# Second FFN's input: blocked loads, gate scaling on GpSimd and 32x32 turns on VectorE in place of TensorE products with the identity

## The reference

```python
def _moe_ref(x, w_gate, w1, w2):            # x: 3072 rows of 512
    logits = x @ w_gate                     # 8 experts
    expert_idx = np.argmax(logits, axis=1)
    probs = softmax(logits); gate_w = probs[np.arange(N), expert_idx]
    for e in range(8):                      # rows of expert e
        out[mask] = gate_w[mask, None] * (np.maximum(x[mask] @ w1[e], 0.0) @ w2[e])

def _moe2_ref(x, w_in, w_out, a, b):        # 512 -> 2048 -> 512
    h = x @ w_in
    P = a[0] + a[1] * h + a[2] * h**2 + a[3] * h**3
    Q = 1.0 + np.abs(b[0]) * np.abs(h) + np.abs(b[1]) * h**2
    return (P / (Q + 1e-06)) @ w_out
```

## Time and profile before

| | before |
|---|---|
| median of 3 runs | 1113.38 us (1112.99 to 1115.29) |
| the profiled execution | 1118.07 us, span 1116.4 us |
| TensorE busy | 1088.4 us, 97% |
| VectorE busy | 921.7 us, 83% |
| ScalarE busy | 593.2 us, 53% |
| GpSimd busy | 259.6 us, 23% |
| granted TensorE clock | 0.996 |

### The profile page before, as it was taken

One profiled execution on the slowest core, in us unless ns is written; L12 is line 12 of the kernel. 1 busy time (PEld: TensorE's weight loads), 2 busy tenths in 40 slices (PEclk: granted clock), 3 DMA queues, 4 the chain that ended last, 5 costly groups with the idle time before them and its releaser, 6 DMA issues.

```text
span 1116.4 us, 19594 instructions
## 1 busy us (share of the span) xinstructions
PE 1088.4 (97%) x5911; PEld 878.1 (79%) x5912; DVE 921.7 (83%) x1844; ACT 593.2 (53%) x1060; POOL 259.6 (23%) x191
## 2 busy tenths in 40 slices
PE   6999999899999999999999999999999999999997
PEld 4777777678888888888787888888888888888885
DVE  5788888759898989898859979977986986987975
ACT  6878888322323232323257556556655665655663
POOL 1022111255756666564300002002001002000101
PEclk9999999999999999999999999999999999999999
DMA  8999771288877978796531010010001002000000
GB/s 200 251 288 262 175 204 50 72 249 298 273 237 262 313 224 282 252 294 219 179 98 38 1 39 38 1 39 38 0 31 45 0 0 72 5 0 10 29 1 38
DMA packets 155754, 142.52 MB, mean 128 GB/s; under 512 B 106160, under 2 KB 122032, under 8 KB 154672
## 3 DMA queue, kind: packets, MB, share of 16 engines
q0 software_dynamic: 27584, 92.48, 24.2%
q1 hardware_dynamic: 127824, 49.19, 17.6%
q10 hardware_dynamic: 288, 0.13, 0.0%
HBM read 118.70 MB, written 23.32 MB: 127 GB/s over the span
## 4 chain that ended last, share of the span: by engine, by line
PE 70%; DVE 8%; DMA 1%; ACT 1%; issue 1%; POOL 0%; POOLq 0%; ACTq 0%; DVEq 0%
PE bank L1177 23%; PE bank L1178 23%; PE bank L1179 23%; DVE bank L1704 1%; DVE poly L1800 1%; DVE poly L1798 1%; PE bank L1249 1%; DVE poly L1813 1%; DVE gl L1822 1%; DMA routed_x<-xt,slot_now 0%; DVE quot_a L1792 0%; DVE quot_a L1816 0%; DVE quot_a L1807 0%; DVE w_lo L1768 0%; DVE quot_b L1816 0%
## 5 line engine op out<-in xcount | busy, mean ns | idle before, releaser
L1704 DVE STREAM_TRANSPOSE bank<-hbuf 32x256 f32<-32x256 f32 x464 | 211.5, 456 | 28.7 <-ACT hbuf L781 22.2
L499 POOL TENSOR_TENSOR w_lo<-stage,w_hi 128x2048 fp32r<-128x2048 f32 x32 | 147.6, 4614 | 66.4 <-DMA w_hi<-in_moe_w_dram 32.6
L1177 PE MATMUL bank<-w_hi,gh 128*128 128x512 f32 x384 | 150.5, 392 | 0.3 <-DVE gl L1822 0.3
L1177 PE MATMUL bank<-x2Th,w_hi 128*128 128x512 f32 x384 | 149.5, 389 | 0.5 <-DVE poly L1800 0.5
L1179 PE MATMUL bank<-w_hi,gl 128*128 128x512 f32 x384 | 149.5, 389 | 0.0
L1178 PE MATMUL bank<-w_lo,gh 128*128 128x512 f32 x384 | 149.4, 389 | 0.0
L1179 PE MATMUL bank<-x2Th,w_lo 128*128 128x512 f32 x384 | 149.4, 389 | 0.0
L1178 PE MATMUL bank<-x2Tl,w_hi 128*128 128x512 f32 x384 | 149.4, 389 | 0.0
L635 POOL DMA_INDIRECT out_dram<-stage,ids x24 | 29.6, 1235 | 510.1 <-ACT stage L895 494.4
L1177 PE MATMUL bank<-w_hi,xTh 128*128 (+1 forms) x240 | 97.1, 405 | 0.8 <-DVE xTl L1610 0.8
L1178 PE MATMUL bank<-w_lo,xTh 128*128 (+1 forms) x240 | 94.2, 392 | 0.0
(11 more groups left out here) (228 smaller groups left out, 2225.8 us busy)
## 6 DMA issues: line engine op xcount, KB each, us to landing
w_hi<-in_moe_w_dram POOLq DMA_DIRECT2D x32, 1024.0 KB, 7.8
stage<-in_moe_w_dram POOLq DMA_DIRECT2D x32, 1024.0 KB, 8.2
routed_y<-ybuf SPq DMA_DIRECT2D x31, 256.0 KB, 3.4
xg<-routed_x SPq DMA_DIRECT2D x122, 64.0 KB, 5.1
x<-routed_y SPq DMA_DIRECT2D x6, 1056.0 KB, 5.1
kraw<-in_k_dram SPq DMA_DIRECT2D x24, 256.0 KB, 4.8
qraw<-in_q_dram SPq DMA_DIRECT2D x24, 256.0 KB, 4.5
vraw<-in_v_dram SPq DMA_DIRECT2D x24, 256.0 KB, 3.9
```

The costliest lines, as they stand in the source:

```text
L499: pool.tensor_tensor(w_lo[:, at:at + CH], stage[:, c % 2, :], w_hi[:, at:at + CH].bitcast(F32), ALU.subtract).then_inc(chunk_ready, 1)
L1177: pe.matmul(dst, lhs_hi, rhs_hi, start=first, stop=False)
L1704: ins = dve.transpose(HB_ps[k][r * QD:(r + 1) * QD, :, q % 2 * QD:(q % 2 + 1) * QD], rows)
```

## The change

- `load_x2` now issues nine transfers a group in place of one. Four bring 32 partitions of `x2` each: partition 32a + n holds, for each of 16 blocks b of 32 rows, 128 numbers of row 32b + n. Four bring the logits to the same four quarters, so each gate is computed in all four. One brings the token numbers (`idf`). The load of the next group waits for the turns on VectorE and for the token numbers to be taken over.
- `moe_y` writes `ybuf` in another order of its columns, so that the four quarters of a stored row are what the four quarters of partitions need.
- The gate work runs on 128 partitions by 16 by 8 rather than by 4 by 8.
- The multiplication by the gate is one instruction over 128x2048 with the gate as second operand. For group 0 VectorE does it (`scale_first`), for groups 1 to 5 GpSimd (`scale_x2`), ahead of the scatter of the group before.
- TensorE's turns go. VectorE turns each half with one 32x32-block transpose of 128x1024, for group 0 into `x2f` (where `x2Tl` will stand), for the others at the ends of steps 5 and 6 into the unused half of `stage`. `x2_high` and `x2_low` read there.
- At the end of the expert stage ScalarE does `gate_exp(0)` after `moe_h` and `moe_x`, and VectorE does `moe_ht` of the last but one tile before the gate work.
- `up` waits for `poly_ready` from step 0 on in later groups, since the turn that held that wait is gone.

The core of the diff:

```diff
+        x2t = [stage[:, k, CH // 2:CH].rearrange("p (j n) -> p j n", j=2) for k in range(2)]
+        x2f_half = [x2f[:, 2 * k:2 * k + 2, :] for k in range(2)]
             def load_x2(g):
-                sp.dma_start(x2[:, :, :], ys[ds(g * G * P, G * P), :].rearrange("(j p) n -> p j n", p=P)).then_inc(x2_in, 16)
+                rows = ds(g * G * P, G * P)
+                for a in range(4):
+                    own = slice(a * QD, (a + 1) * QD)
+                    sp.dma_start(glog[own, :, :], ys[rows, DM:TOK].rearrange("(b n) e -> n b e", n=QD)).then_inc(x2_in, 16)
+                    sp.dma_start(x2[own, :, :], ys[rows, a * P:(a + 1) * P].rearrange("(b n) c -> n b c", n=QD)).then_inc(x2_in, 16)
+                sp.dma_start(idf[:, :, :], ys[rows, TOK:RW].rearrange("(j p) o -> p j o", p=P)).then_inc(x2_in, 16)
...
-            with pool.Fori(0, NG) as g:
+            def scale_x2(g):
+                pool.wait_ge(g_step, 3 * (g + 1))
+                settle(pool)
+                pool.tensor_tensor(x2[:, :, :], x2[:, :, :],
+                                   gate[:, 3, :].rearrange("p (b o) -> p b o", o=1).broadcast_to([P, G * P // QD, P]),
+                                   ALU.mult).then_inc(x2_scaled, 1)
...
+            with pool.Fori(0, NG - 1) as g:
+                scale_x2(g + 1)
+                scatter(g)
+            scatter(NG - 1)
...
-            gate_exp(0)
-            act_tile(MT - 2)
+            moe_h(MT - 2); moe_x(MT - 1); gate_exp(0); moe_y(MT - 3); moe_ht(MT - 2)
             moe_h(MT - 1)
-            x2_high(0, 0, first_ps)
             end_ht(2, hLh)
+            x2_high(0, 0, x2f_half[0])
+            x2_high(0, 1, x2f_half[1])
+            moe_y(MT - 2)
             split_high(0)
             split_high(1)
-            moe_y(MT - 2)
-            x2_high(0, 1, first_ps)
...
-            turn_x2(0, 0, first_ps)
             turn_end_h(MT - 1)
             moe_down(MT - 2, off_down, e_down)
-            turn_x2(0, 1, first_ps)
             moe_down(MT - 1, off_last, e_last, YL_ps, hLh, hLl)
...
-                if p >= 2:
+                if p >= 2 or later(g):
                     pe.wait_ge(poly_ready, n - 1)
...
-                    if p == PAIRS - 1 and not last:
-                        turn_x2(g + 1, 0, pair_ps[0])
                     if p >= 2:
                         down(g, p - 2, again)
-                if not last:
-                    turn_x2(g + 1, 1, pair_ps[1])
...
-                for j in range(G):
-                    ins = dve.tensor_scalar(x2[:, j, 0:DM], x2[:, j, 0:DM], gate[:, 3, j:j + 1], None, ALU.mult)
-                ins.then_inc(x2_scaled, 1)
+            def turn_x2(g, k, dst):
+                dve.wait_ge(x2_scaled, g + 1)
+                dve.transpose(dst.rearrange("p j (b n) -> p j b n", n=QD),
+                              x2[:, :, 2 * k * QD:2 * (k + 1) * QD].rearrange("p b (j n) -> p j b n", n=QD)).then_inc(x2_turned, 1)
...
                     if not last and p == 4:
-                        gate_scale(g + 1)
+                        gate_sum(g + 1)
+                    if not last and p in (5, 6):
+                        turn_x2(g + 1, p - 5, x2t[p - 5])
```

More of the change, by code:

```diff
@@ L166, in build_program @@
         x2_at = free[1]
-        x2 = over("x2", [P, G, RW])
+        x2 = over("x2", [P, G * P // QD, P])
+        glog = over("glog", [P, G * P // QD, E])
+        gate = over("gate", [P, 4, G * P // QD])
+        idf = over("idf", [P, G, RW - TOK])
         xSh, x2_at = place("xSh", [P, KB, P], F32R, x2_at)
@@ L170, in build_program @@
         x2Th = over("x2Th", [P, KB, G * P], F32R)
+        x2f, _ = place("x2f", [P, KB, G * P], F32, free[1])
         x2Tl = over("x2Tl", [P, KB, G * P], F32R)
@@ L1728, in _, with gate_sum @@
             turn_rows(MT - 1, 0, MT // 2 + 1)
+            per_row = lambda k, n: gate[:, k, :].rearrange("p (b o) -> p b o", o=1).broadcast_to([P, G * P // QD, n])
             def gate_shift(g):
[L1732 to L1733 removed]
+                dve.wait_ge(x2_in, 144 * (g + 1))
+                dve.tensor_reduce(gate[:, 0, :], glog[:, :, :], AX.X, ALU.max).then_inc(g_shift, 1)
                 dve.wait_ge(g_shift, 2 * g + 1)
[L1735 to L1740, removed]
+                dve.tensor_tensor(glog[:, :, :], glog[:, :, :], per_row(0, E), ALU.subtract).then_inc(g_shift, 1)
+                dve.tensor_copy(ids[:, 1, :], idf[:, :, 0]).then_inc(ids_next, 1)
+            def gate_sum(g):
                 dve.wait_ge(g_exp, g + 1)
@@ L1746, in gate_scale, with scale_first @@
                 dve.reciprocal(gate[:, 3, :], gate[:, 2, :]).then_inc(g_step, 1)
-                dve.wait_ge(g_step, 3 * g + 3)
-                for j in range(G):
-                    ins = dve.tensor_scalar(x2[:, j, 0:DM], x2[:, j, 0:DM], gate[:, 3, j:j + 1], None, ALU.mult)
-                ins.then_inc(x2_scaled, 1)
+            def scale_first():
+                dve.wait_ge(g_step, 3)
+                dve.tensor_tensor(x2[:, :, :], x2[:, :, :], per_row(3, P), ALU.mult).then_inc(x2_scaled, 1)
+            def turn_x2(g, k, dst):
+                dve.wait_ge(x2_scaled, g + 1)
+                dve.transpose(dst.rearrange("p j (b n) -> p j b n", n=QD),
+                              x2[:, :, 2 * k * QD:2 * (k + 1) * QD].rearrange("p b (j n) -> p j b n", n=QD)).then_inc(x2_turned, 1)
             def take_ids(g):
@@ L1771, in _ @@
             gate_shift(0)
-            turn_h(MT - 2, 0); moe_x(MT - 1); turn_h(MT - 2, 1)
-            gate_scale(0)
-            moe_ht(MT - 2)
-            x2_low(0, 0, first_ps)
+            turn_h(MT - 2, 0); moe_x(MT - 1); turn_h(MT - 2, 1); moe_ht(MT - 2)
+            gate_sum(0)
+            scale_first()
+            turn_x2(0, 0, x2f_half[0])
             end_ht(MT - 1, hLh, hLl)
+            turn_x2(0, 1, x2f_half[1])
+            x2_low(0, 0, x2f_half[0])
+            x2_low(0, 1, x2f_half[1])
             split_low(0)
             split_low(1)
-            x2_low(0, 1, first_ps)
             CE = 1.0 + 1e-6
@@ L1851, in group @@
                     if p == PAIRS - 1:
-                        x2_low(g + 1, 0, pair_ps[0])
-                        x2_low(g + 1, 1, pair_ps[1])
+                        x2_low(g + 1, 0, x2t[0])
+                        x2_low(g + 1, 1, x2t[1])
                     quotient(g, p)
```

29 lines of the change are left out of this document (9 added, 20 removed).

## The result

The changed kernel took 1127.46 us (median of 4 runs, 1126.78 to 1129.12), the kernel before 1113.18 on the same chip: 14.3 us slower, ratio 1.0127 [1.0114, 1.0139]. The forecast was 1123.2, the range ended at 1127.0. So the direction was right and the size too small: +14.3 for +9.8. All later runs are compared with runs of the kernel before on their own chip, as a ratio with its 95% interval.

A forecast was written before the change was run, and what follows sets the result against it. At the seam between groups the chain ScalarE to VectorE, ending at g_low(6), was taken as a bound beside TensorE, without slack. Terms -3.0 + 5.9 + 6.9 = +9.8 on 1113.4 gave 1123.2 us, range 1110.0 to 1127.0.

The forecast's parts named there:

- The seam of groups 1 to 4: Ahead of down(g, 6): a wait for g_low(6) of 1.75 us replaces TensorE's two turns, gain 0.
- TensorE is the bound after all: Rival, chance 0.10: g_low(6) comes earlier without the turns, each of five seams gives 1.7 us; sum -11.5, 1101.9 us.
- The start, -3.0: End of the expert stage up to up(0, 0): relus sooner -0.8, turns gone and fewer waits -2.2; bounds 0 and -4.4.
- Group 0, +5.9: VectorE without a pause from step 4 to g_low(6), so every us counts: 0.45 - 1.58 + 4.6 + 1.2 + 1.2.
- 0.45 - 1.58: VectorE: larger gate work around steps 3 and 4 adds 0.45 us, the four removed multiplications save 1.58.
- 4.6 + 1.2 + 1.2: VectorE in group 0: 4.6 us held by GpSimd's multiplication, plus two transposes of 128x1024 at 1.2 us each.
- the holding: Step 5: GpSimd's multiplication gets in behind den(5) and holds VectorE's g_low(4) for 4.6 us; bounds 0 and 4.6.
- Groups 1 to 4, +6.9: VectorE 2.94 us late at step 6, 1.7 at step 7, so g_low(6), down(6) and each group 1.7 late.
- To step 6: 0.45 - 1.58 + 4.6 + 1.2 = 4.67, less 1.73: Groups 1 to 4: gates, removed multiplications, GpSimd's 4.6 us and a transpose, less VectorE's idle time: 2.94 us late.
- Loads, 0 up to +2: Nine transfers read some 50 us after issue: 0, up to +2 us for the first, issued among the expert stage's row loads.

The follow-up runs named there:

- seam_addr: addr_back with step 7 in the order of the other steps (g_low(6) ahead of the numerator): 1110.06 us, ratio 0.9948 to the kernel before.
- addr_back: The changed kernel with two unused gaps that put w_hi, x2Th and x2Tl back on multiples of 256 bytes: 1123.31 us, ratio 1.0069 to the kernel before.
- no_scale: The changed kernel with GpSimd's multiplication by the gate in groups 1 to 5 replaced by a signal alone: 1125.5 us, ratio 1.008 to the kernel before.
- addr_moved: The kernel before with an unused gap of 448 bytes behind x2, so x2Th starts at 198848: 1122.94 us, ratio 1.0066 to the kernel before.
- pool_only: The kernel before plus, in groups 0 to 4, a 128x2048 GpSimd subtraction nobody waits for: 1119.67 us, ratio 1.0041 to the kernel before.
- best: seam_addr with the gate's multiplication on VectorE at the end of step 4, as in dve_scale: 1108.42 us, ratio 0.9932 to the kernel before.
- dve_scale: addr_back with the gate's multiplication as one VectorE instruction at the end of step 4, GpSimd only signalling: 1120.42 us, ratio 1.0043 to the kernel before.

## Why the prediction was right and where it was wrong

The time came out above the range because the sum lacked the placement (6.5 us) and the half rate behind the pause (2.0) and held too little for the first load (some 5 us for up to 2), while its term for groups 1 to 4 was 6.9 us too large.

- *The seam of groups 1 to 4: right.* I forecast a wait of 1.75 us in place of two turns, gain 0; the wait is 1.58. seam_addr shows that the chain to g_low(6) was what bound it, since the gain comes as soon as that chain is shorter. The rival "TensorE is the bound after all" fell.
- *The start, -3.0: right.* From one fixed product of the expert stage (474.98 in addr_back, 476.79 before) to up(0, 0) are 95.47 us in addr_back, whose trace has no wait for the load, and 98.35 before: -2.9.
- *Group 0, +5.9: the mechanism right, a term too large.* From up(0, 0) to down(0, 6) 84.17 us for 79.87, +4.3. To den(5) it is 56.92 for 58.00, -1.1 (forecast 0.45 - 1.58). From there to the start of g_low(6) it is 25.98 for 20.59, +5.4, where I had 4.6 + 1.2 + 1.2 = 7.0. A transpose came to 1.16. The mis-sized term is the holding: g_low(4) took 4.63 - 1.22 = 3.4 more. I had priced GpSimd's instruction by the earlier trace rows, but alone it takes 3.61, not 4.61. The row was of another operation that also writes fp32r; same size was not same price. I had also read from the earlier trace rows that GpSimd's transfers go in ahead of VectorE's next instruction. The next ones, at 763.40 and 769.30, take their usual 1.22 us, so those rows show GpSimd waiting for VectorE and nothing of the reverse.
- *Groups 1 to 4, +6.9: wrong.* The holding costs nothing there in the changed kernel (no_scale: the same 90.24), and 0.35 per group with fast products. The step that failed is "To step 6: 0.45 - 1.58 + 4.6 + 1.2 = 4.67, less 1.73". It lets the whole 4.6 us of GpSimd fall behind den(5). But once the four multiplications are gone, den(5) waits 1.15 us for ScalarE, and GpSimd's 3.61 us begin in that wait, so 2.4 us are left to hold. From the start of the reciprocal to the end of den(5) are 5.13 us, before 3.08: 2.0 late, where the sum had 3.0. With 0.45 for the gates and two transposes of 1.16 that is 4.8 against the 4.15 of idle time, or at most 0.7 us late at step 7, an estimate from these rows. addr_back shows 0.35. In the changed kernel nothing is left of it; there each block of up is 0.15 us longer, which gives VectorE time, but that this absorbs it is argued and not tested.
- *Placement: a missing term, +6.5 (1.3 us in each of groups 1 to 5).* I had looked at which instructions the change moves and not at where it moves the tiles.
- *The clock after a pause: a missing term, +2.0.* I had priced the pause of group 0 and not what follows it.
- *Loads, 0 up to +2: too small.* They cost about 5 us in the profiled execution (100.68 us from the fixed product to up(0, 0), for 95.47 in addr_back) and nothing visible in others. I had counted the transfers' time and not the 8.1 to 9.9 us that their issues hold SyncE, nor the stores behind them.

Together: 4.3 + 6.5 + 2.0 = +12.8 from up(0, 0) to the end, and the two traces have 554.11 us for 541.30, which is the same. With the start that is +9.9 without the wait for the load, and some 15 with it. Measured: +14.3 on the first chip, and 0.0094 x 1113.3 = +10.5 on the second, where three of four executions seem to have been without it. So +9.8 came near the truth for a part of the executions for a wrong reason: 6.9 us of holding that are not there stood in for 6.5 us of placement.

## What to carry to other kernels

When a change adds or removes tiles, work out the byte addresses of what TensorE reads before and after, and time one block of products in both traces from its first start to the next block's. Here a shift of x2Th and what lies behind it cost as much as any wait, and a shift of w_hi cost nothing visible. A kernel with the old addresses settles it. A GpSimd instruction beside VectorE's is paid for where VectorE has no idle time, even if nobody waits for its result. Before work is taken off the engine that looks like the bound, see which chain ends at its next product, and shorten that one along with it.

## What the runs showed of the hardware

- Products of 128x512 that stream x2Th and x2Tl start every 0.2267 us with these at multiples of 256 bytes (before, addr_back) and every 0.233 with them, and the tiles behind them, at odd multiples of 64 (the change, addr_moved). Products that stream w_hi and w_lo start every 0.227 at either kind of address. Only these addresses were tried, so the rule stays open.
- After a pause TensorE ran some products at a start-to-start time of 0.43 us, and how many does not follow from the pause alone. After 4.6 to 4.8 us it was 8 to 14, from the first one on (six traces). After 2.51 us it was seven (pool_only). After 2.33 us it was eight in best, from the seventh product on, and none in seam_addr. After 2.07 us it was none (no_scale). After 1.92 us it was eight or nine at two of four seams of addr_back and none at the other two. After 1.58 us it was none, at all 24 seams of six traces.
- GpSimd's multiplication of 128x2048 with a factor per row takes 3.61 us alone, its subtraction with fp32r output 4.61, and one in f32 on one tile 3.72 (pool_only).
- SyncE's issues of loads with short rows took 0.4 to 0.5 us at first and up to 2.9 once some were under way, up to 3.5 in dve_scale and seam_addr.
